# Contraction over all 128 rows in a DFT stage, another order of transposes and first loads, and a table moved out of the folding buffer

## What is computed

```python
def phi(x):                                   # attention: 4 batches, 8 heads, 576 tokens, 64 channels
    proj = np.einsum('bhsd,df->bhsf', x, w_phi)                # 128 features
    proj = proj - np.max(np.abs(proj), axis=-1, keepdims=True)
    return np.concatenate([np.exp(proj), np.exp(-proj)], axis=-1)
kv, z = einsum('bhsf,bhsd->bhfd', phi(k), v), phi(k).sum(axis=2)
x = einsum('bhsf,bhfd->bhsd', phi(q), kv) / (einsum('bhsf,bhf->bhs', phi(q), z) + 1e-6)
# first block, x is (4, 576, 512)
u = x + np.real(fft(fft(x, axis=1), axis=2))  # over tokens, then over channels
x = u + relu(layernorm(u) @ w_ch1) @ w_ch2    # 512 -> 2048 -> 512
# second block: token MLP (576 -> 256 -> 576), then channel MLP (512 -> 1536 -> 512)
```

## Time and profile before

| | |
|---|---|
| median of 3 runs | 1012.19 us (1010.32 to 1013.43) |
| the profiled execution | 1010.74 us, its span 1008.9 us |
| PE busy | 993.0 us, 98% of the span |
| DVE, ACT, POOL busy | 38%, 29%, 19% |
| granted TensorE clock | 1.0 of full in all 40 slices |
| the 16 pair steps | end at 211.27 us |

### The profile page before, as it was taken

How to read it: one execution, slowest core, us unless ns; L and a number is a source line. 1 busy time by engine, 2 the same in 40 slices (tenths; PEclk the granted TensorE clock), 3 DMA queues, 4 the chain that set the end, 5 groups by cost and what they waited for, 6 DMA issues and landing times.

```text
span 1008.9 us, 17341 instructions
## 1 busy us (share of the span) xinstructions
PE 993.0 (98%) x7299; PEld 881.8 (87%) x7299; DVE 379.5 (38%) x746; ACT 289.8 (29%) x577; POOL 186.8 (19%) x161
## 2 busy tenths in 40 slices
PE   7989999999999999999999999999999999999998
PEld 5988989878899999999899999768999899999897
DVE  5897878862331321322313213463121212121211
ACT  5865756554411111111111112252111111111110
POOL 4554555269800000000000000045000000000000
PEclk9999999999999999999999999999999999999999
DMA  6322231434400010010010200685010000000000
GB/s 207 95 84 65 76 121 52 135 116 152 152 33 31 1 63 1 1 62 0 16 46 0 83 20 1 198 302 198 1 46 18 34 30 32 31 31 31 19 13 32
DMA packets 47854, 66.29 MB, mean 66 GB/s; under 512 B 22640, under 2 KB 23600, under 8 KB 47664
## 3 DMA queue, kind: packets, MB, share of 16 engines
q1 hardware_dynamic: 46064, 59.10, 17.9%
q10 hardware_dynamic: 1728, 6.29, 1.7%
HBM read 46.51 MB, written 18.87 MB: 65 GB/s over the span
## 4 chain that ended last, share of the span: by engine, by line
PE 89%; DVE 5%; POOL 4%; issue 1%; ACT 1%; DMA 0%; SPq 0%; DVEq 0%; POOLq 0%; ACTq 0%
PE mlp_hid L1028 11%; PE mlp_y L1043 11%; PE mlp_hid L1030 11%; PE mlp_y L1044 11%; PE mlp_hid L1029 11%; PE mlp_y L1042 11%; PE kv L317 3%; PE num L331 2%; PE proj L288 2%; PE four L342 2%; POOL mlp_w_lo L990 1%; PE mlp_turn_in L1013 1%; PE proj L290 1%; PE proj L289 1%; DVE pm L621 1%; DVE absmax L613 1%
## 5 line engine op out<-in xcount | busy, mean ns | idle before, releaser
L1146 DVE SCALAR_TENSOR_TENSOR mlp_h_lo<-mlp_hid,mlp_h_hi 128x384 fp32r<-128x384 f32 x168 | 93.7, 558 | 465.7 <-ACT mlp_h_hi L1078 465.7
L1028 PE MATMUL mlp_hid<-mlp_ut_hi,mlp_w_hi 128*128 128x384 f32 x672 | 229.4, 341 | 1.2 <-POOL mlp_w_lo L990 0.5
L1078 ACT ACTIVATE mlp_h_hi<-mlp_hid 128x384 fp32r<-128x384 f32 x168 | 82.7, 492 | 505.5 <-PE mlp_hid L1030 505.5
L1030 PE MATMUL mlp_hid<-mlp_ut_hi,mlp_w_lo 128*128 128x384 f32 x672 | 226.5, 337 | 0.0
L1029 PE MATMUL mlp_hid<-mlp_ut_lo,mlp_w_hi 128*128 128x384 f32 x672 | 225.4, 335 | 0.0
L1044 PE MATMUL mlp_y<-mlp_w_hi,mlp_h_lo 128*128 128x512 f32 x504 | 199.4, 396 | 0.0
L1043 PE MATMUL mlp_y<-mlp_w_lo,mlp_h_hi 128*128 128x512 f32 x504 | 198.9, 395 | 0.0
L1042 PE MATMUL mlp_y<-mlp_w_hi,mlp_h_hi 128*128 128x512 f32 x504 | 197.1, 391 | 0.4 <-DVE mlp_h_lo L1146 0.2
L990 POOL TENSOR_TENSOR mlp_w_lo<-mlp_w_raw,mlp_w_hi 128x1024 fp32r<-128x1024 f32 x26 | 61.7, 2390 | 403.3 <-DVE tok_x_lo L1381 380.8
L1028 PEld LDWEIGHTS mlp_hid<-mlp_ut_hi,mlp_w_hi 128*128 128x128 f32 x672 | 126.3, 188 | 7.7 <-DVE mlp_ut_lo L1132 1.3
L1029 PEld LDWEIGHTS mlp_hid<-mlp_ut_lo,mlp_w_hi 128*128 128x128 f32 x672 | 126.3, 188 | 5.3
(11 more groups left out here) (127 smaller groups left out, 1099.8 us busy)
## 6 DMA issues: line engine op xcount, KB each, us to landing
mlp_u<-u_scratch SPq DMA_DIRECT2D x12, 768.0 KB, 4.5
mlp_w_raw<-in_w_mlp SPq DMA_DIRECT2D x14, 512.0 KB, 4.5
mlp_w_raw<-in_w_mlp ACTq DMA_DIRECT2D x12, 512.0 KB, 4.9
v<-in_v SPq DMA_DIRECT2D x16, 320.0 KB, 3.6
qk<-in_kT SPq DMA_DIRECT2D x16, 288.0 KB, 4.0
qk<-in_qT SPq DMA_DIRECT2D x16, 288.0 KB, 4.0
u_scratch<-x_all SPq DMA_DIRECT2D x4, 1024.0 KB, 4.8
x_scratch<-mlp_u SPq DMA_DIRECT2D x5, 768.0 KB, 3.6
```

Source lines behind the costliest of these rows:

```text
L1028: nc.tensor.matmul(out, w_hi[:, j, col], hi, start=(c == 0), stop=False)
L1030: last = nc.tensor.matmul(out, w_lo[:, nf - 1 - j, col], hi, start=False, stop=(c == DC - 1))
L1078: nc.scalar.activation(h_hi[:, j % 2, :], hid[j % 2][:, 0:BT], ACT.Relu).then_inc(h_rounded, 1)
L1146: nc.vector.scalar_tensor_tensor(out=h_lo[:, j % 2, :], in0=hid[j % 2][:, 0:BT], scalar=0.0, in1=h_hi[:, j % 2, :], op0=ALU.max, op1=ALU.s ...
```

## The change

1. **128 rows.** All slabs of the s pieces contract 128 rows; the rows beyond 33 or 32 hold zeros. The one-row chunk of the spectrum gets its low part at partition 32 of `ab_hi` (its other rows are cleared), and the table row is repeated there; so one matmul of 128 rows takes the place of the two of one row.
2. **Transposes.** `pe_turn` 0 goes ahead of REST, `pe_turn` 2 directly behind `pe_kv`.
3. **First loads.** Keys of pair 0 come first, then 64 columns of queries, wphi, the other queries; then pair 1, the identity and v. Pair 0's low parts are made on VectorE in two pieces (640 and 512 columns) instead of on GpSimd. Pair 1 is rounded earlier on ScalarE. WARM goes from 15 to 11.
4. **Table.** The raw table lies in x's third slot, which is cleared after step 2; the folds of pairs 0, 1, 2 need not wait for it and are made in steps 1, 2, 3.

```diff
-    table = at("table", [128, 2 * FRONT * D], F32, 81920)
+    table = at("table", [128, TCOLS], F32, 24576)
+    fold_flat = at("fold", [128, 2 * FRONT * D], F32, 81920)
...
     def ready(k):
-        if k == 3:
-            return [0, 1, 2]
-        return [k - 1] if k > 3 else []
+        return [k - 1] if k > 0 else []
...
     def sync(sp):
-        sp.dma_start(wphi[:, :], dram["wphi"]).then_inc(consts_loaded, 16)
-        sp.dma_start(ident_a[:, :], dram["ident"]).then_inc(consts_loaded, 16)
-        load_qk(sp, Pair(0))
+        sp.dma_start(qk[:, 0, KEY], dram["kT"][0]).then_inc(k_loaded[0], 16)
+        sp.dma_start(qk[:, 0, S:S + TAIL], dram["qT"][0][:, 0:TAIL]).then_inc(tail_loaded, 16)
+        sp.dma_start(wphi[:, :], dram["wphi"]).then_inc(wphi_loaded, 16)
+        sp.dma_start(qk[:, 0, S + TAIL:], dram["qT"][0][:, TAIL:]).then_inc(q_loaded[0], 16)
+        load_qk(sp, Pair(1))
+        sp.dma_start(ident_a[:, :], dram["ident"]).then_inc(ident_loaded, 16)
         load_v(sp, Pair(0))
-        load_qk(sp, Pair(1))
         load_v(sp, Pair(1))
-        sp.dma_start(table[:, 0:TCOLS], dram["table"]).then_inc(table_loaded, 16)
         load_qk(sp, Pair(2))
+        sp.dma_start(table[:, :], dram["table"]).then_inc(table_loaded, 16)
...
     def pe_over_s(pe, b, c, out_bank):
-            deep = 128 if t else ROWS[2] + (1 if cosine else 0)
-            last = passes(out, fold_hi[0:deep, k, t, first:first + rows], ...
+            last = passes(out, fold_hi[:, k, t, first:first + rows], ...
     def pe_cosines(pe, b, m, out_bank):
-        for c in range(3):
-            k = 128 if c < 2 else 1
-            ...
+        for c in range(2):
+            passes(out, ab_hi[:, c, cols], ab_lo[:, c, cols], table_hi[:, col], table_lo[:, col], c == 0, False)
+        last = nc.tensor.matmul(out, ab_hi[:, 2, cols], table_hi[:, TALT:TALT + FREQ], start=False, stop=True)
...
     def pe_step(pe, k):
         for s in range(5):
+            if k >= 0 and s == 0:
+                pe_turn(pe, p, 0)
             if following < PAIRS:
                 pe_project(pe, Pair(following), s)
             for b, i in pieces_in(k, s):
                 pe_piece(pe, b, i)
             if k >= 0:
-                if s == 0:
-                    pe_turn(pe, p, 0)
                 if s == 2:
                     pe_turn(pe, p, 1)
                     pe_kv(pe, p)
+                    pe_turn(pe, p, 2)
                 if s == 3:
-                    pe_turn(pe, p, 2)
...
     def scalar(act):
-        act.wait_ge(consts_loaded, 32)
+        act.wait_ge(tail_loaded, 16)
+        act.wait_ge(k_loaded[0], 16)
+        nc.scalar.copy(qk_hi[:, 0, 0:S + TAIL], qk[:, 0, 0:S + TAIL]).then_inc(qk_rounded, 1)
+        act.wait_ge(wphi_loaded, 16)
         nc.scalar.copy(wphi_hi[:, :], wphi[:, :]).then_inc(wphi_rounded, 1)
-        act_round(act, Pair(0), KEY)
-        act_round(act, Pair(0), QUERY)
+        act.wait_ge(q_loaded[0], 16)
+        nc.scalar.copy(qk_hi[:, 0, S + TAIL:], qk[:, 0, S + TAIL:]).then_inc(qk_rounded, 1)
+        act_round(act, Pair(1), KEY)
...
     def vector(dve):
+        nc.vector.memset(ab_hi[:, 2, :].bitcast(F32), 0.0).then_inc(ab_cleared, 1)
...
+        dve.wait_ge(qk_rounded, 1)
+        nc.vector.tensor_tensor(qk_lo[:, 0, 0:S + TAIL], ..., ALU.subtract).then_inc(qk_split, 1)
         dve.wait_ge(wphi_rounded, 1)
         nc.vector.tensor_tensor(wphi_lo[:, :], wphi[:, :], wphi_hi[:, :], ALU.subtract).then_inc(wphi_split, 1)
+        dve.wait_ge(qk_rounded, 2)
+        nc.vector.tensor_tensor(qk_lo[:, 0, S + TAIL:], ..., ALU.subtract).then_inc(qk_split, 1)
```

More of the change, by code:

```diff
@@ L105, in front @@
     row288 = at("row288", [1, D], F32, 155776)
-    folds = table[:, :].rearrange("p (k t d) -> p k t d", k=2, t=FRONT)
+    folds = fold_flat[:, :].rearrange("p (k t d) -> p k t d", k=2, t=FRONT)
     fold_s, fold_d = folds[:, 0], folds[:, 1]
@@ L187, in front @@
     TAIL = S - 512
+    LOW_ROW = 32
     FIRST = {KA: 0, KB: 256, REST: 512, QA: 512 + 2 * TAIL, QB: 768 + 2 * TAIL}
-    WARM = 15
+    WARM = 11
     LAST = B - 1
@@ L279, in pe_project @@
     def pe_project(pe, p, unit):
-        if unit == REST:
+        if p.n == 0 and unit in (REST, QA):
+            pe.wait_ge(qk_split, 1 if unit == REST else 2)
+        elif unit == REST:
             pe.wait_ge(qk_split, 2 * p.n + 2)
@@ L342, in passes @@
         nc.tensor.matmul(out, lhs_hi, rhs_hi, start=start, stop=False)
-        if rhs_lo is not None:
-            nc.tensor.matmul(out, lhs_hi, rhs_lo, start=False, stop=False)
+        nc.tensor.matmul(out, lhs_hi, rhs_lo, start=False, stop=False)
         return nc.tensor.matmul(out, lhs_lo, rhs_hi, start=False, stop=stop)
@@ L369, in pe_over_s @@
         for t in range(FRONT):
-            deep = 128 if t else ROWS[2] + (1 if cosine else 0)
             col = slice(base + step * t, base + step * t + n)
-            last = passes(out, fold_hi[0:deep, k, t, first:first + rows], fold_lo[0:deep, k, t, first:first + rows],
-                          table_hi[0:deep, col], table_lo[0:deep, col], t == 0, t == FRONT - 1)
+            last = passes(out, fold_hi[:, k, t, first:first + rows], fold_lo[:, k, t, first:first + rows],
+                          table_hi[:, col], table_lo[:, col], t == 0, t == FRONT - 1)
         last.then_inc(s_done, 1)
@@ L380, in pe_cosines @@
         cols = slice(128 * m, 128 * m + rows)
-        for c in range(3):
-            k = 128 if c < 2 else 1
-            col = slice(TDC + FREQ * c, TDC + FREQ * c + FREQ) if c < 2 else slice(TALT, TALT + FREQ)
-            last = passes(out_bank[0:rows, 0:FREQ], ab_hi[0:k, c, cols], ab_lo[0:k, c, cols], table_hi[0:k, col],
-                          table_lo[0:k, col] if c < 2 else None, c == 0, c == 2)
+        out = out_bank[0:rows, 0:FREQ]
+        for c in range(2):
+            col = slice(TDC + FREQ * c, TDC + FREQ * c + FREQ)
+            passes(out, ab_hi[:, c, cols], ab_lo[:, c, cols], table_hi[:, col], table_lo[:, col], c == 0, False)
+        last = nc.tensor.matmul(out, ab_hi[:, 2, cols], table_hi[:, TALT:TALT + FREQ], start=False, stop=True)
         last.then_inc(d_done, 1)
@@ L512, in act_piece @@
                 wait_if(act, d_done, 2 * FRONT * b)
+            if at_ == 2 and b == 0:
+                act.wait_ge(ab_cleared, 1)
             nc.scalar.copy(ab_hi[0:rows, at_, 0:n], four_bank(b, i)[0:rows, 0:n]).then_inc(s_rounded, 1)
@@ L630, in dve_norm @@
         b, column = p.n // 4, (p.n % 4) * (2 * DH)
-        if p.n == 0:
-            dve.wait_ge(x_cleared, 2)
+        if p.n in (0, 8):
+            dve.wait_ge(x_cleared, 2 if p.n == 0 else 4)
         if b >= SLOTS and p.n % 4 == 0:
@@ L648, in dve_sum @@
         dve.wait_ge(x_done, p.n + 1)
-        if b == 0:
-            dve.wait_ge(table_split, 3)
-        else:
+        if b > 0:
             dve.wait_ge(fold_split, 2 * b - 1)
@@ L678, in dve_piece @@
             dve.wait_ge(s_rounded, 5 * b + at_ + 1)
-            nc.vector.tensor_tensor(ab_lo[0:rows, at_, 0:n], four_bank(b, i)[0:rows, 0:n], ab_hi[0:rows, at_, 0:n],
+            low = ab_hi[LOW_ROW:LOW_ROW + 1, 2, 0:n] if at_ == 2 else ab_lo[:, at_, 0:n]
+            nc.vector.tensor_tensor(low, four_bank(b, i)[0:rows, 0:n], ab_hi[0:rows, at_, 0:n],
                                     ALU.subtract).then_inc(s_split, 1)
@@ L761, in pool_fold @@
             pool.wait_ge(fold_split, 2 * b)
-        else:
-            pool.wait_ge(table_split, 3)
         x = x_of(b)
@@ L806, in pool_step @@
                                     ALU.subtract).then_inc(table_split, 1)
+        if k == 2:
+            pool.wait_ge(table_split, 3)
+            for tile in (0, 5):
+                nc.gpsimd.memset(x_all[:, 2, tile, :], 0.0).then_inc(x_cleared, 1)
         if k == PAIRS - 1:
@@ L1563, in constants @@
         table[:, TDS + FREQ * c:TDS + FREQ * c + D // 2] = np.sin(angle)[:, :D // 2]
-    table[0, TALT:TALT + D // 2 + 1] = (-1.0) ** kd
+    table[0:64:32, TALT:TALT + D // 2 + 1] = (-1.0) ** kd
     return table.astype(np.float32), np.eye(128, dtype=np.float32)
```

22 lines of the change are left out of this document (14 added, 8 removed).

## The result

| | before | changed |
|---|---|---|
| median of the timed executions, us | 1012.15 (4) | 998.30 (4) |
| lowest and highest, us | 1010.32, 1013.43 | 998.04, 998.75 |
| profiled execution, us | 1010.74 | 998.43 |
| its span, us | 1008.9 | 996.6 |

The ratio of the times is 0.9865, with a 95% interval of 0.9848 to 0.9882: faster, by 13.9 us in the medians and by 12.3 us in the spans of the two profiled executions.

The account below looks back on a forecast made before the run. PE work was taken as 89% of the chain of waits. Terms -3.2 + 3.0 - 2.35 - 8.3 - 0.9 = -11.75 gave 999.0 from the profiled 1010.74, and 1000.5 from the 1012.19 median; range 995.5 to 1005.

Parts of the forecast that it names:

- Start and pair 1: Kernel start through pair 1: earlier keys and low parts on VectorE, PE beginning at 6.9; -3.2 us (2.0 to 4.3).
- or at 0.75 (that term 1.3 better): Sign at the start: activation table load at 0.75, not behind the keys' landing, would make the start term 1.3 better.
- The transposes: Pair steps: transposes ahead of REST make PE wait 0.45 us before KB where no piece covers it; +3.0 (0 to 4.5).
- 6 x 0.45 + 3 x 0.1: Sum for the transposes' wait before KB, with less in steps 5, 9, 13 where VectorE is late already; +3.0 us.
- The table: Step 3 loses two extra folds, -2.35 us; steps 1 and 2 take them under cover of VectorE's idle time.
- 128 rows: s and cos pieces: row-count switches and one cos matmul go, 2.8 us a batch; -8.3 us for three batches.
- The rival that 128 rows save only the matmuls that go: Switches come with every new piece, not from row count; total about -4, time 1008 us; chance 0.12.
- the 0.1 put against step 15: Deduction of 0.1 us from the three batches' saving, since ScalarE's copies come last in step 15.
- The last batch: Behind the front: PE's 2.8 us saving is waited away, only GpSimd's wait for a row copy shortens; -0.9 (0 to 2.8).
- The wait before KB does not come: Rival in the pair steps: transposes ahead of REST cause no PE wait; 3.0 better, 997.5 us; chance 0.12.
- the loss at the MLP's start: Rival where the MLP begins: weight loads or GpSimd don't move along; half the front's gain lost, 1006 us; chance 0.06.
- The ring through QA: Rival in the steps: transposes wait for QA's subtraction, so REST and VectorE's next step slip; 1014 us, slower; chance 0.04.

Follow-up runs that it names:

- the table's part alone: Kernel before with only the raw tables in x's third slot and folds of pairs 0, 1, 2 in steps 1, 2, 3: 1010.63 us, ratio 0.9984.
- the kernel with 100 rows: Changed kernel with slab 0 of the s pieces contracting 100 rows, the others 128: 998.23 us.
- The experiment with the last batch alone: Changed kernel with 33 and 32 rows in the s pieces of the last batch only: 998.29 us.
- the kernel with 33 rows: Changed kernel with slab 0 of the s pieces back at 33 and 32 contracted rows, cos pieces keeping 128: 1003.94 us.
- The kernel with 64 rows: Changed kernel with slab 0 of the s pieces contracting 64 rows: 1003.61 us.

## Why the prediction was right, and where its steps were not

**The forecast.** 1000.5 was predicted and 998.3 measured, inside the range. Against the profiled execution the sum was −11.75 and the spans give −12.3. Most of the miss of the median is not in the sum but in its last line, "for the median of after I subtract from it": it takes for granted that median and profiled execution differ by the same thing before and after. The 1.45 us between them fit two falls of the clock, which cost 1.7 us of span in the one execution that was profiled with them; both stand at standstills that the change removes. The other executions show only their mean clock, so for them this is inferred. Both standstills stood in the rows, the start's in the list of waits, step 3's as the 2.3 us in which PE is not busy there; that they could cost more than their own length in other executions was not considered.

**Start and pair 1.** −3.2 predicted, −3.45 measured; PE at 7.01 (6.9), first maximum at 7.77 (7.5). Right in size, wrong in one link: the table load was taken to be on the path and the prediction's own mark, "or at 0.75 (that term 1.3 better)", fails: at 0.75 it is worth nothing until the late query columns are off VectorE.

**The transposes.** +3.0 predicted, +0.7 to +0.8 measured. The mechanism is there: measured by starts, as the prediction does, PE's wait before KB grew from 0.05 to 0.50 (34.05 to 34.67, less 0.12), the 0.45 that was put; the profile writes 0.34 because it counts from the modelled end of the last matmul. A step grows by less, 0.35 to 0.4: KB comes 1.65 behind REST as before, and the transposes ahead of REST take 0.40 (32.62 to 33.02). The step that failed is the sum "6 x 0.45 + 3 x 0.1". Steps 3 and 4 (in it at 0.45) and 5, 9 and 13 cost nothing, because VectorE was late there in the old order too; what is left is 4 x 0.35, less what the group behind `kv` gives in step 3 (0.6) and plus what it costs in step 15 (0.3).

**The table.** −2.35 predicted; step 3 has lost 2.0 with the new wait of 0.34 inside it, so the length is as put. The term's size depends on the company: worth 3.2 us in the changed kernel, of which 2.1 are step 3 and the rest is only in part explained by a fall of the clock, and 1.85 alone in the old one, with a fall of the clock in it. That "VectorE is busy some 8.2 of 9.6 us" covers a fold held: steps 1 and 2 grew by the transposes' 0.35 and nothing else, and with the table's part alone they are 9.60 and 9.58 long.

**128 rows.** −8.3 predicted. The s pieces give 5.0 (3 x 1.65 predicted) and the cos pieces 2.3 in the steps or 2.7 in the medians (3.5 predicted), 7.3 to 7.7 in all. Step 6 lost 1.71 (1.6 predicted), step 7 0.69 (0.85). The rival that 128 rows save only the matmuls that go is out: the kernel with 100 rows has the same number of matmuls as those with 33 and 64, and is 5.4 us faster. What failed is the 0.1 put against step 15, which by the prediction should have lost about 0.75 and grew by 0.39. Two things stand behind it.

First, the second transposes wait for ScalarE. The rows from 187.63 on of the changed kernel's timeline, in the section on the result, show the chain: VectorE's statistics for the first MLP group, ScalarE's root, another table load and then the exponentials stand ahead of them. Before, the root ran 0.84 us behind the start of step 15 (200.38 against 199.54) and PE did not wait; now it runs 1.23 behind (188.99 against 187.76). That is not because step 14 became 1.7 us shorter: with 33 rows in the s pieces step 14 is 16.32 long, 1.3 more than in the changed kernel, and the root still runs 1.24 behind. With the cos pieces put back, it runs 0.92 behind, and PE waits 0.16 instead of 0.62. So what PE saves in the cos pieces, the one at the end of step 14 above all, stands there as a wait.

Second, this wait alone does not lengthen the step: with both groups of transposes in their old places it is 0.85 us, and step 15 is 11.79 long, 0.06 more than before. The other 0.33 came with the second group of transposes, now behind `kv` (12.13 with only the first group back). The piece behind it then comes later, so do ScalarE's copies of that piece and the copy of `kvs` behind them, and PE stands still 0.28 us before the `num` matmuls that read `kvs`. The prediction priced this move at 0. In the trace the profile names no releaser for that wait ("issue"); that it is the copy is read from the order of ScalarE's program and the times, not tested alone.

**The last batch.** −0.9 predicted, −0.9 measured, by the way that was put: GpSimd's wait of 0.94 us for the row is gone (223.92). The experiment with the last batch alone confirms that what PE saves in its s pieces is worth nothing, and GpSimd's wait stays away there too. Mis-sized was PE's part. From the end of step 15 to the matmul that waits for `mlp_w_lo` it takes 43.1 us instead of 44.1, with 2.5 us of standstills in it instead of 1.4; so PE's own work shrank by 2.0 us and not by 2.8, and the wait for `mlp_w_lo` grew by 0.4, not by 2, the wait of 0.49 before a piece being new.

**The other rivals.** "The wait before KB does not come" and the loss at the MLP's start are out by the rows above. The ring through QA did not form: steps 1 to 4 are 9.94 or 9.95 each.

Added up, the transposes and the table came out 1.3 better in their nine steps than put, the start 0.25 better, and steps 6, 7, 10, 11, 14 and 15 together 1.1 worse: −11.75 − 0.45 = −12.2. The misses of the terms nearly cancelled, which is luck and not method.

## What to carry to other kernels

Price a wait only in the steps in which the engine behind it is not already late for another reason: ask of each step what ends last there, and put beside each other what runs beside each other. Read the granted clock and the span of every timed execution, not only of the profiled one; standstills of TensorE of 2.3 and 2.5 us cost 0.9 to 2.5 us beyond their own length here, and the one profile may not show it. Matmuls of 64 rows or fewer in a stream of 128-row ones are worth padding with zeros (0.18 us for each change here), unless the stretch has another engine's chain at its end.

## What the runs showed of the hardware

The granted clock fell at standstills of 2.03 to 2.54 us, but not in every execution: behind 2.52, 2.55 and 2.28 us in the first profile of the kernel before it stayed at 1.00, behind 2.54 and 2.29 in the second it fell to 0.50 for some three microseconds each time, and at the 2.54 of the kernel with the table's part alone for nearly seven. These three cost 1.4, 0.9 and 2.5 us. In no profile of a kernel with the new start and the spread folds is a window of 1 us below 1.00 while PE works (one has 0.67 at 994 to 995, behind the last matmul).

The start has a second uncertainty, which the granted clock doesn't show. In the kernel with 33 rows the windows from 7 to 11 us say 1.00, while the projections there start 0.21 us apart, the pace of the 1.2 GHz level, until about 10.2 us (7.48 to 7.70 in the rows of the experiment); in the changed kernel they start 0.12 apart from the second on. That cost 0.9 us at the end of step 0. The kernel with 64 rows shows the same, and the one with the table's load freed has it for its first 0.6 us; why the high pace came later in these executions stays open.
